# The first layer's attention tiles written out, each with its own order of scores, products, sums and x

## The chip, the cores and the metric

One core of a Trainium2 chip. The metric is device time in microseconds of one execution; lower is better. The engines: TensorE (PE: matmuls and transposes, with its weight loads as PEld), VectorE (DVE), ScalarE (ACT), GpSimd (POOL) and SyncE (SP), on whose queue all of this kernel's loads and stores are issued.

## What is computed

```python
# q, k, v: (B=4, H=8, S=576, D=64), float32
q_d, k_d, v_d = (t.reshape(B, H, 144, 4, D).mean(axis=3) for t in (q, k, v))
out_up = np.repeat(softmax(scale * q_d @ k_d.T) @ v_d, 4, axis=2)
mask = np.abs(pos[:, None] - pos[None, :]) < 4
out_local = softmax(np.where(mask, scale * q @ k.T, -1e9)) @ v
x = (out_up + out_local) as (B * S = 2304, H * D = 512)
h = x @ w_in                          # first layer, 512 -> 2048 -> 512
x = (h * sigmoid(h)) @ w_out
r = np.maximum(x @ w2_in, 0)          # second layer, same sizes
return (s * r * r + b) @ w2_out
```

Each query sees seven keys locally, and 144 pooled keys.

## The kernel before

**Tiles.** Every matmul of the two layers is made of three, of the high and low parts of both operands. The first layer goes over N1 = 8 tiles of T1 = 288 rows (half a batch each). Tile t has 32 blocks of 12 matmuls: "up" f (512 to 128 of the 2048 columns) and "down" f. They are dealt out in 8 slots of 4 blocks (48 matmuls, counted as places k = 0 to 47). Slot 0 has up 0, up 1, up 2, down 0; slot u has up 2u+1, down 2u-1, up 2u+2, down 2u; slot 7 has up 15, down 13, 14, 15. Behind an up block stand ACT's tanh (L880), VectorE's gate (L1152), ACT's high part (L836) and GpSimd's low part (`g_low`, L320). Down f waits for the low part of f.

**Attention beside it.** During tile t the attention of the half that tile t+1 needs is prepared; tile 0 and the time ahead of it work otherwise and are not changed. A unit is one head of one half: 8 per half. TensorE puts a unit's parts between its blocks: scores (L587, L590; the local ones and the pooled ones), transposes of the pooled probabilities `prob_d` (L614), and the matmuls on the pooled values (`attend`, L635). Between these stand VectorE's `maxima` (L1081, L1084), ACT's `exps` (L844, and a copy of the local scores into `s_sb`), VectorE's `normalise` (L1103 to L1107) and `pT_copy` (L1122), and ACT's `evacuate`. GpSimd makes the pooled keys (`qk_sums`, L1436 and L1440) and the pooled values (`v_sums`, L1451 and L1455), both once for two units. In SyncE's queue, per unit: `load_qk` and `load_v` for later units, `read_band` of the unit before, and `store_band`, which waits for the unit's exps. Before each tile stand the windows of v (`load_windows`, four transfers), which wait for the last sum of the tile before.

**Local part by rows.** The stored bands of a half's 8 units come back as rows of seven scores (`e_rows`). In the softmax slot VectorE and ACT make `p_rows` of them. Then for each of 9 groups of rows a product with the windows of v goes into one of two buffers (`weigh`: GpSimd L1497, and VectorE L1263 for i = 2, 5, 8), and VectorE reduces it (`sum_row`, L1273). Product i waits for sum i-2, by these lines:

```python
if not (isinstance(n, int) and n < 2):
    gp.wait_ge(rows_summed, n - 1)
```

Three sums at a time are transposed on TensorE (`turn`, L677), and ACT copies them (`place`). When the third turn is placed, VectorE adds the pooled part for each of four chunks (`x_add`, L1283), ACT rounds (`x_round`) and GpSimd takes the rest (`x_low`); the next tile's up 0 waits for each chunk (`x1_ready`). The local scores, the transposes and the turns share two banks of PSUM with what ACT evacuates.

**Order.** All orders are written by hand in the tables at the top and in each engine's `slot_rows`. `UNITS` says which unit's scores are in which slot, as a count on from the half's first: the lead is 7 units in tiles 2 to 6, while tile 1 makes 14 units (two in each of slots 0 to 5). Tiles 2 to 5 are a loop (`Fori`, two turns of two tiles) on every engine; tiles 1, 6 and 7 are straight code. In tile 6 only the half's last unit is left to finish. Tile 7 has no attention, and the second layer follows.

## Time and profile before

| | |
|---|---|
| median of three runs | 1015.57 us (1011.75 to 1016.58) |
| the profiled execution | 1015.92 us, its span 1014.1 us |
| mean granted clock of TensorE | 0.981 |
| TensorE busy | 956.6 us, 94% of the span |
| VectorE, ACT, GpSimd busy | 474.0, 365.2, 431.7 us |
| tiles 1 to 6 of the first layer | from 113.9 to 563.5 us of the span |
| tile 7 and the second layer | from 563.5 us on |

The span is from the first to the last instruction of one profiled execution. A busy TensorE is not TensorE at its peak: matmuls overlap, their ends are modelled, and they take twice as long where the granted clock is half. The clock's column is 1.00 at 2.4 GHz and 0.50 at 1.2 GHz. Idle time of another engine costs nothing unless TensorE waits for it.

### The profile page before, as it was taken

Reading aid. Unit: us, or ns where it says so; the run is one execution under the profiler, and the core shown is the slowest. Engines: PE = TensorE matmul, PEld = TensorE weight load, DVE = VectorE, ACT = ScalarE, POOL = GpSimd, SP = SyncE. Lnnn points to the kernel's source line nnn. Section 1 sums busy time; section 2 is a strip of 40 time slices with the busy share of each in tenths; the row PEclk is TensorE's granted clock in tenths of the full one; section 3 lists DMA queues with packets and bytes.
Section 4 is the critical chain, followed back from the end, with each engine's and each line's share of the span. In section 5 each row is a group of like instructions: output and inputs, shape, how many; then the busy total and the mean of one; then the engine's idle time right before and its main releaser. Section 6 shows DMA issues by size and latency. Waiting matters only on the chain.

```text
span 1014.1 us, 16827 instructions
## 1 busy us (share of the span) xinstructions
PE 956.6 (94%) x6071; PEld 874.1 (86%) x6071; DVE 474.0 (47%) x975; ACT 365.2 (36%) x951; POOL 431.7 (43%) x426
## 2 busy tenths in 40 slices
PE   8999997788998978998999999999999999999998
PEld 8899987777988977998999998888888888888897
DVE  5577434656747726647638465223222322322232
ACT  5665432232343332443333564223222322322232
POOL 6678355645555645555646322221322222222222
PEclk9899999889999989999999999999999999999999
DMA  6555444133152142152130554002000200100010
GB/s 184 156 166 144 101 108 102 29 79 98 45 117 65 41 108 71 45 133 48 41 73 1 158 167 131 8 1 73 11 0 1 83 0 0 62 0 0 0 43 22
DMA packets 87179, 68.85 MB, mean 68 GB/s; under 512 B 38720, under 2 KB 73024, under 8 KB 87104
## 3 DMA queue, kind: packets, MB, share of 16 engines
q1 hardware_dynamic: 87104, 67.86, 25.0%
q8 instruction: 46, 0.75, 0.3%
q14 instruction: 29, 0.24, 0.1%
HBM read 52.76 MB, written 15.08 MB: 67 GB/s over the span
## 4 chain that ended last, share of the span: by engine, by line
PE 65%; issue 13%; POOL 11%; DVE 6%; ACT 2%; DMA 1%; POOLq 0%; SPq 0%; ACTq 0%; DVEq 0%
PE pH L797 19%; PE pY L812 19%; PE pH L737 11%; PE pY L742 8%; POOL weighted L1497 3%; POOL g_hl L320 3%; PE pS L587 2%; POOL vd_f L1451 2%; POOL pair L1436 1%; POOL x_hl L320 1%; DMA stage_in<-w_in 1%; PE pS L590 1%; DVE act L1152 1%; DVE g_gap L1273 1%; PE pO L641 1%
## 5 line engine op out<-in xcount | busy, mean ns | idle before, releaser
L320 POOL TENSOR_TENSOR g_hl<-act,g_hl 128x288 fp32r<-128x288 f32 (+2 forms) x208 | 203.0, 976 | 504.5 <-ACT g_hl L836 504.5
L737 PE MATMUL pH<-x_hl,w_in_hl 128*128 128x288 f32 x1518 | 250.2, 306 | 11.4 <-POOL x_hl L320 5.0
L742 PE MATMUL pY<-g_hl,w_out_hl 128*128 128x288 f32 x1536 | 249.4, 302 | 2.2 <-POOL g_hl L320 2.2
L737 PEld LDWEIGHTS pH<-x_hl,w_in_hl 128*128 128x128 f32 x1518 | 216.8, 193 | 15.9 <-POOL x_hl L320 8.6
L742 PEld LDWEIGHTS pY<-g_hl,w_out_hl 128*128 128x128 f32 x1536 | 216.1, 190 | 3.6 <-POOL g_hl L320 3.6
L797 PE MATMUL pH<-x_hl,w_in_hl 128*128 128x512 f32 (+1 forms) x960 | 208.4, 368 | 0.0
L812 PE MATMUL pY<-w_out_hl,g_hl 128*128 128x512 f32 x864 | 207.8, 390 | 0.0
L797 PEld LDWEIGHTS pH<-x_hl,w_in_hl 128*128 128x128 f32 x960 | 169.0, 188 | 31.0
L812 PEld LDWEIGHTS pY<-w_out_hl,g_hl 128*128 128x128 f32 x864 | 161.2, 188 | 33.2 <-POOL g_hl L320 0.3
L836 ACT ACTIVATE g_hl<-act 128x288 fp32r<-128x288 f32 (+2 forms) x208 | 104.1, 500 | 229.1 <-DVE act L1152 125.3
L1384 DVE TENSOR_TENSOR act<-act 128x512 f32<-128x512 f32 (+1 forms) x80 | 55.5, 694 | 270.6 <-ACT act L1056 270.6
L1056 ACT ACTIVATE act<-pH 128x512 f32<-128x512 f32 (+1 forms) x80 | 44.3, 554 | 166.0 <-PE pH L797 165.7
L880 ACT ACTIVATE act<-pH 128x288 f32<-128x288 f32 x128 | 52.1, 407 | 135.9 <-PE pH L737 135.8
L1152 DVE SCALAR_TENSOR_TENSOR act<-act,pH 128x288 f32<-128x288 f32 x128 | 57.4, 448 | 63.0 <-ACT act L880 62.1
L1497 POOL TENSOR_TENSOR weighted<-p_rows,v_loc 128x896 f32<-128x896 f32 x36 | 60.8, 1689 | 23.0 <-DVE p_rows L1254 18.0
L1273 DVE TENSOR_REDUCE g_gap<-weighted 128x128 f32<-128x896 f32 x36 | 63.3, 1760 | 11.4 <-POOL weighted L1497 11.0
L587 PE MATMUL pS<-qk_f 128*96 128x102 f32 x360 | 45.3, 264 | 7.0 <-POOL d_f L1440 7.0
L587 PEld LDWEIGHTS pS<-qk_f 128*96 128x96 f32 x360 | 41.5, 174 | 8.8 <-POOL d_f L1440 8.8
L1451 POOL TENSOR_TENSOR vd_f<-vd_f 72x512 f32<-72x512 f32 x32 | 40.8, 1275 | 18.2 <-DMA vd_f<-vp 18.2
L844 ACT ACTIVATE pS<-pS,stats 72x144 f32<-72x144 f32 x60 | 20.8, 346 | 68.6 <-DVE stats L1084 52.6
L1386 DVE TENSOR_SCALAR act<-act,sb_col 128x512 f32<-128x512 f32 (+1 forms) x80 | 41.6, 520 | 2.9
L614 PE MATMUL pO<-ident,prob_d 72*72 72x72 f32 x120 | 18.9, 240 | 23.2 <-ACT g_gap L836 12.4
(141 smaller groups left out, 821.1 us busy)
## 6 DMA issues: line engine op xcount, KB each, us to landing
qk_f<-qk SPq DMA_DIRECT2D x32, 292.0 KB, 3.5
vd_f<-vp SPq DMA_DIRECT2D x64, 144.0 KB
stage_in<-w_in SPq DMA_DIRECT2D x32, 256.0 KB, 2.9
stage_out<-w_out SPq DMA_DIRECT2D x32, 256.0 KB, 3.0
v_loc<-vp SPq DMA_DIRECT2D x24, 240.0 KB, 4.9
score_bands<-act SPq DMA_DIRECT2D x48, 114.8 KB, 2.5
qk_f<-qk SPq DMA_DIRECT2D x64, 72.0 KB, 3.0
x_scratch<-y_sb SPq DMA_DIRECT2D x8, 576.0 KB, 4.8
```

What stands on the lines that cost most here:

```text
L320: eng.tensor_tensor(lo, full, hi.bitcast(F32), ALU.subtract).then_inc(signal, 1)
L587: pe.matmul(work(n).s_loc[:, j, :], qk_f[:, buf, q0:q0 + TQ], qk_f[:, buf, c:c + KW], start=not masked_by_pe(n) and j == 0, stop=True, ski ...
L737: last = pe.matmul(pH[:, f % 2, 0:T1], w_in[:, wp, c, f * P:(f + 1) * P], x1[:, par, mp, c, :], start=c + n == 0, stop=c == C - 1 and n == 2)
L742: last = pe.matmul(pY[:, c, 0:T1], w_out[:, wp, f, c * P:(c + 1) * P], g_hl[:, f % RING, mp, 0:T1], start=f + n == 0, stop=f == NF - 1 and ...
L797: last = pe.matmul(pH[:, f % 2, 0:T], w_in[:, wp, c, f * P:(f + 1) * P], x2_hl[:, xp, c, 0:T], start=c + n == 0, stop=c == C - 1 and n == 2)
L812: last = pe.matmul(pY[:, j, :], g_hl[:, f % RING, gp, j * P:(j + 1) * P], w_out[:, wp, f, :], start=f + n == 0, stop=f == NF - 1 and n == 2)
L836: return sc.activation(dst, src, ACT.Copy)
L1152: ve.scalar_tensor_tensor(act1[:, f % RING, :], act1[:, f % RING, :], 1.0, pH[:, f % 2, 0:T1], ALU.add, ALU.mult).then_inc(L[0].g_ready, 1)
L1273: ve.tensor_reduce(o_row[i].rearrange("p (h d) -> p h d", h=2), weighted[:, i % 2].rearrange("p (h r d) -> p h d r", h=2, r=NR), AX.X, ALU ...
L1384: ve.tensor_tensor(g, g, g, ALU.mult).then_inc(squared, 1)
L1451: gp.tensor_tensor(src[:, :, 0:2, :], src[:, :, 0:2, :], src[:, :, 2:4, :], ALU.add).then_inc(vpair_summed, 1)
L1497: gp.tensor_tensor(*weigh_operands(i), ALU.mult).then_inc(weighed_by_pool, 1)
```

## The change

The loop over tiles 2 to 5 is gone: tiles 1 to 6 are written out on all engines, and tables give tiles 1 and 2 orders of their own. Tile 1 makes units 1 to 12 (two in each of slots 0 to 3), tile 2 makes 5 to 14 (two in slots 0 and 1); from tile 3 on it is 7 to 14, as before. All nine products of a tile are on GpSimd. Sums, counted by slot in `SUM`, are no longer in the slots of their products: one stands at the head of a slot, the others at its end. In GpSimd's slots two products stand ahead of everything else (in the softmax slot they stand behind), the key sums stand behind the first low part of the slot, and the value sums behind them. In slots with two units, maxima stand ahead of the gate, and exps ahead of the high part. The last turn is at place 6 of slot 7 instead of 14 (tile 1: two turns in slot 7, at 6 and 47). In slot 7 `x_add` 0 is ahead of the gate and the rounding of x ahead of the unit's exps. TensorE waits for the copies of turns (`bank_placed`) ahead of the transposes also, and a turn waits for what holds the bank at its place.

```diff
@@ -53,18 +53,21 @@
 LEAD = 7
 UNITS = [(u + LEAD,) for u in range(H)]
-FIRST_UNITS = [(1, 2), (3, 4), (5, 6), (7, 8), (9, 10), (11, 12), (13,), (14,)]
-
+UNITS_IN = {1: [(1, 2), (3, 4), (5, 6), (7, 8), (9,), (10,), (11,), (12,)],
+            2: [(5, 6), (7, 8), (9,), (10,), (11,), (12,), (13,), (14,)]}
+
+SOFTMAX, SOFTMAX_IN = 2, {1: 5, 2: 3}
 WEIGH = {2: (0, 1), 3: (2, 3), 4: (4, 5), 5: (6, 7), 6: (8,)}
-FIRST_WEIGH = {5: (0, 1, 2), 6: (3, 4, 5), 7: (6, 7, 8)}
-BY_VECTOR = (2, 5, 8)
-BY_POOL = tuple(i for i in range(TB) if i not in BY_VECTOR)
+WEIGH_IN = {1: {5: (0, 1, 2), 6: (3, 4, 5), 7: (6, 7, 8)}, 2: {3: (0, 1), 4: (2, 3, 4), 5: (5, 6), 6: (7, 8)}}
+SUM = {2: (0,), 3: (1, 2), 4: (3, 4), 5: (5, 6), 6: (7, 8)}
+SUM_IN = {1: {5: (0, 1), 6: (2, 3, 4, 5), 7: (6, 7, 8)}, 2: {3: (0,), 4: (1, 2), 5: (3, 4, 5), 6: (6, 7, 8)}}
+QK_AHEAD = {(1, 9): 0, (2, 9): 0, (1, 12): 2}
 GROUP = 3
-TURNS = {(4, 24): 0, (6, 24): 1, (7, 14): 2}
-FIRST_TURNS = {(6, 24): 0, (7, 12): 1, (7, 42): 2}
-
-ONE_UNIT, LAST_UNIT, FIRST_LAST_UNIT = (9, 15, 38), (3, 20, 38), (3, 18, 47)
-TWO_UNITS = (3, 7, 19), (27, 31, 43)
+TURNS = {(4, 24): 0, (6, 24): 1, (7, 6): 2}
+TURNS_IN = {1: {(6, 24): 0, (7, 6): 1, (7, 47): 2}, 2: {(5, 24): 0, (6, 24): 1, (7, 6): 2}}
+
+ONE_UNIT, LAST_UNIT, FIRST_LAST_UNIT = (9, 15, 38), (18, 22, 40), (18, 22, 36)
+TWO_UNITS = (4, 7, 20), (28, 31, 44)
...
@@ -468,21 +471,22 @@
                     sp.wait_ge(wout_ready, NF)
                     load_windows((2, 0, 1))
-                def tile1(t, h, following):
-                    ahead = 3 if isinstance(t, int) and t == 1 else 1
+                def tile1(t, following):
+                    h = prepared(t)
                     for u in range(H):
-                        for k in units(t, u):
-                            if ahead == 1 or len(units(t, u)) == 1:
+                        now = units(t, u)
+                        for k in now:
+                            if len(now) == 1:
+                                if w := unit(h, k + QK_AHEAD.get((t, k), 1)):
+                                    load_qk(w)
                                 if w := unit(h, k + 1):
-                                    if k != FIRST_UNITS[-2][0] or ahead == 1:
-                                        load_qk(w)
                                     load_v(w)
                             if w := unit(h, k - 1):
                                 read_band(w)
                             if w := unit(h, k):
                                 store_band(w)
-                            if ahead == 3 and len(units(t, u)) == 2:
-                                load_qk(unit(h, k + 3))
+                            if len(now) == 2 and (w := unit(h, k + 3)):
+                                load_qk(w)
                                 load_v(unit(h, k + 1))
                         if u == 1:
...
                     last.then_inc(rows_turned, 1)
-                def placed(t, u, k):
-
-                    before = [g for (slot, at), g in turns(t).items() if slot == u and at < k]
-                    if before:
-                        pe.wait_ge(rows_placed, TB // GROUP * (t - 1) + max(before) + 1)
+                def bank_placed(t, u, k):
+
+                    before = [g for (slot, at), g in turns(t).items() if (slot, at) < (u, k)]
+                    if t > 1 or before:
+                        pe.wait_ge(rows_placed, TB // GROUP * (t - 1) + len(before))
                 def small_rows(t, h, u, k):
...
@@ -691,17 +688,27 @@
                     elif u < H - 1:
                         places = ONE_UNIT,
                     else:
-                        places = (FIRST_LAST_UNIT if isinstance(t, int) and t == 1 else LAST_UNIT),
+                        places = (FIRST_LAST_UNIT if late(t, u) else LAST_UNIT),
                     for v, (at_trans, at_scores, at_attend) in zip(now, places):
-                        if k == at_trans:
-                            trans_unit(unit(h, v - 1))
+                        before = unit(h, v - 1)
+                        if k == at_trans and before:
+                            bank_placed(t, u, k)
+                            trans_unit(before)
                         if k == at_scores:
                             score_unit(unit(h, v))
                         if (u, k) in turns(t):
-                            turn(t, turns(t)[u, k], unit(h, v - 1))
-                        if k == at_attend and unit(h, v - 1):
-                            placed(t, u, k)
-                            attend_unit(unit(h, v - 1))
+                            if not before:
+                                pe.wait_ge(o_copied, H * (HALVES - 1))
+                            elif k < at_trans:
+                                pe.wait_ge(o_copied, before[0] - H)
+                            elif k < at_attend:
+                                pe.wait_ge(pT_copied, before[0] + 1)
+                            else:
+                                pe.wait_ge(o_copied, before[0] - H + 1)
+                            turn(t, turns(t)[u, k])
+                        if k == at_attend and before:
+                            bank_placed(t, u, k)
+                            attend_unit(before)
                 def up1(t, par, f, c, fill=False):
                     if fill and c == 0:
@@ -778,11 +785,8 @@
                     if u < H - 1:
                         keep_warm(WARM_SOFTMAX)
                 tile1(0, 0, (1, 1, 0), fill=True, rows=False)
-                tile1(1, 1, (2, 0, 1))
-                with pe.Fori(0, B - 2) as i:
-                    tile1(2 * i + 2, 0, halves(i, 0))
-                    tile1(2 * i + 3, 1, halves(i, 1))
-                tile1(N1 - 2, 0, (HALVES - 1, 1, B - 1))
+                for t in range(1, N1 - 1):
+                    tile1(t, t % 2, prepared(t))
                 tile1(N1 - 1, 1, None)
...
@@ -967,38 +971,44 @@
                 def slot_rows(t, h, u):
                     now = units(t, u)
-                    last = u == H - 1
                     here = groups(t, u)
-                    if w := unit(h, now[0] - 2):
+                    two = len(now) == 2
+                    if (w := unit(h, now[0] - 2)) and not (u == 0 and late(t - 1, H - 1)):
                         evacuate(w)
                     if u == 1:
                         tanh1(t, CARRIED)
                         g_high(L[0], t, CARRIED, 2, T1)
+                    if u == H - 1:
+                        place(t, h, here[0])
                     if u == 0:
                         y_out1(t - 1)
                     f, more = UPS[u][0], UPS[u][1:]
                     tanh1(t, f)
-                    if last:
-                        place(t, h, here[0])
+                    if two:
+                        exps(unit(h, now[0]))
+                    if u == H - 1 and not late(t, u):
+                        x_round(t, h, 0)
                     g_high(L[0], t, f, 2, T1)
                     if u == softmax_in(t):
                         row_exps(t, h)
-                    if w := unit(h, now[0]):
+                    if u == H - 1 and not late(t, u):
+                        for c in range(1, C):
+                            x_round(t, h, c)
+                    if two:
+                        evacuate(unit(h, now[0] - 1))
+                    elif w := unit(h, now[0]):
                         exps(w)
-                    if len(now) == 2:
-                        evacuate(unit(h, now[0] - 1)) if now[0] > 0 else None
-                    if not last:
+                    if u < H - 1:
                         for g in here:
                             place(t, h, g)
-                    if last and len(here) == 1:
-                        for c in range(C):
-                            x_round(t, h, c)
                     for f in more:
                         tanh1(t, f)
+                    if two:
+                        exps(unit(h, now[1]))
+                    for f in more:
                         g_high(L[0], t, f, 2, T1)
-                    if len(now) == 2:
-                        exps(unit(h, now[1]))
...
                 def sum_row(t, i):
-                    if i in BY_VECTOR:
-                        weigh(t, i)
-                        ve.wait_ge(weighed_by_vector, len(BY_VECTOR) * (t - 1) + BY_VECTOR.index(i) + 1)
-                    else:
-                        ve.wait_ge(weighed_by_pool, len(BY_POOL) * (t - 1) + BY_POOL.index(i) + 1)
-                    if not (isinstance(t, int) and t == 1):
+                    ve.wait_ge(weighed, TB * (t - 1) + i + 1)
+                    if t > 1 and i == 0:
                         ve.wait_ge(rows_turned, TB // GROUP * (t - 1))
                     ve.tensor_reduce(o_row[i].rearrange("p (h d) -> p h d", h=2),
                                      weighted[:, i % 2].rearrange("p (h r d) -> p h d r", h=2, r=NR), AX.X,
...
@@ -1285,38 +1280,44 @@
                 def slot_rows(t, h, u):
                     now = units(t, u)
-                    last = u == H - 1
-                    weighs = weigh_in(t, u)
+                    sums = sum_in(t, u)
+                    two = len(now) == 2
+                    finish = u == H - 1 and not late(t, u)
                     if u == 1:
                         gate1(t, CARRIED)
+                    at_once = 0 if u == softmax_in(t) else 1
+                    for i in sums[:at_once]:
+                        sum_row(t, i)
+                    if finish:
+                        x_add(t, h, 0)
+                        gate1(t, UPS[u][0])
                     if w := unit(h, now[0] - 1):
                         pT_copy(w)
-                    f, more = UPS[u][0], UPS[u][1:]
-                    gate1(t, f)
+                    if two:
+                        maxima(unit(h, now[0]))
+                    if not finish:
+                        gate1(t, UPS[u][0])
                     if u == softmax_in(t):
                         row_normalise(t, h)
-                    if last and len(groups(t, u)) == 1:
-                        for c in range(C):
+                    if finish:
+                        for c in range(1, C):
                             x_add(t, h, c)
-                    if w := unit(h, now[0]):
+                    if not two and (w := unit(h, now[0])):
                         maxima(w)
-                    for i in weighs[:1]:
-                        sum_row(t, i)
                     if w := unit(h, now[0]):
                         normalise(w)
-                    if len(now) == 2:
+                    if two:
                         pT_copy(unit(h, now[0]))
-                    for f in more:
+                        maxima(unit(h, now[1]))
+                    for f in UPS[u][1:]:
                         gate1(t, f)
-                    if len(now) == 2:
-                        maxima(unit(h, now[1]))
-                    for i in weighs[1:]:
+                    if two:
+                        normalise(unit(h, now[1]))
+                    for i in sums[at_once:]:
                         sum_row(t, i)
-                    if len(now) == 2:
-                        normalise(unit(h, now[1]))
                     if u == softmax_in(t) - 1:
                         row_shift(t, h)
-                    if last and len(groups(t, u)) == 2:
+                    if late(t, u):
                         for c in range(C):
                             x_add(t, h, c)
...
@@ -1502,30 +1502,31 @@
                 def slot_rows(t, h, u):
                     now = units(t, u)
-                    last = u == H - 1
-                    weighs = [i for i in weigh_in(t, u) if i in BY_POOL]
+                    two = len(now) == 2
                     if u == 1:
                         g_low(L[0], t, CARRIED, T1)
-                    if len(now) == 2:
+                    if two:
                         qk_sums(unit(h, now[1]))
-                    elif w := unit(h, now[0]):
+                    softmax = u == softmax_in(t)
+                    for i in weigh_in(t, u)[:0 if softmax else 2]:
+                        weigh(t, i)
+                    g_low(L[0], t, UPS[u][0], T1)
+                    if not two and (w := unit(h, now[0] + 1)):
+                        qk_sums(w)
+                    if not two and (w := unit(h, now[0])):
                         v_sums(w)
-                    for i in weighs[:1]:
-                        weigh(t, i)
-                    f, more = UPS[u][0], UPS[u][1:]
-                    g_low(L[0], t, f, T1)
-                    for i in weighs[1:]:
-                        weigh(t, i)
-                    if last and len(groups(t, u)) == 1:
+                    if u == H - 1 and not late(t, u):
                         for c in range(C):
                             x_low(t, h, c)
-                    for f in more:
+                    for i in weigh_in(t, u)[:1 if softmax else 0]:
+                        weigh(t, i)
+                    for f in UPS[u][1:]:
                         g_low(L[0], t, f, T1)
-                    if len(now) == 2:
+                    if two:
                         v_sums(unit(h, now[1]))
-                    elif w := unit(h, now[0] + 1):
-                        qk_sums(w)
-                    if last and len(groups(t, u)) == 2:
+                    for i in weigh_in(t, u)[1 if softmax else 2:]:
```

## Rows read from the trace of the kernel before

**Rows 1.** Tiles 1 to 6: length, busy PE, PEld, DVE, ACT, POOL; clock, DMA.

```profile
113.90:213.50 99.60, 80.93 (x591) 76.69 (x589) 49.47 (x124) 30.95 (x96) 49.34 (x50) 0.92 0.37 85
213.50:286.10 72.60, 66.64 (x505) 64.50 (x505) 44.34 (x88) 26.91 (x77) 41.56 (x43) 0.97 0.28 70
286.10:358.50 72.40, 65.42 (x505) 62.88 (x505) 44.01 (x87) 27.39 (x80) 42.23 (x44) 1.00 0.34 80
358.50:436.70 78.20, 68.33 (x506) 66.25 (x506) 44.01 (x87) 25.73 (x74) 40.45 (x42) 0.93 0.29 71
436.70:508.20 71.50, 65.34 (x505) 62.86 (x506) 44.00 (x87) 26.60 (x77) 41.39 (x43) 1.00 0.33 79
508.20:563.50 55.30, 55.06 (x416) 54.36 (x417) 33.58 (x46) 19.84 (x50) 28.86 (x28) 1.00 0.14 32
```

**Rows 2.** TensorE's waits: us in total, times, longest us.

```profile
PE pO L614 <- ACT g_gap L836: 12.4, 12, 1.9
PE pO L614 <- DVE prob_d L1107: 10.8, 10, 4.4
...
PE pO L677 <- DVE pdT L1122: 2.4, 1, 2.4
```

**Rows 3.** Timeline of TensorE in tile 5: start, us, instructions, idle before.

```profile
453.36 1.49 PE L737 MATMUL pH<-x_hl,w_in_hl 128*128 128x288 f32 x10
...
461.11 1.48 PE L737 MATMUL pH<-x_hl,w_in_hl 128*128 128x288 f32 x10
...
481.80 1.49 PE L737 MATMUL pH<-x_hl,w_in_hl 128*128 128x288 f32 x10
```

**Rows 4.** Timeline of TensorE: the last turn of tile 1; head of tile 4.

```profile
210.18 0.41 PE L677 MATMUL pO<-ident,act 128*128 128x128 f32 x2 [3.62 <-DVE o_last L1273]
...
363.74 0.85 PE L737 MATMUL pH<-x_hl,w_in_hl 128*128 128x288 f32 x2 [3.90 <-issue]
```

**Rows 5.** Timeline of tile 1, TensorE and SyncE's queue.

```profile
119.79 0.78 PE L737 MATMUL pH<-x_hl,w_in_hl 128*128 128x288 f32 x4
...
124.35 0.78 PE L737 MATMUL pH<-x_hl,w_in_hl 128*128 128x288 f32 x4
...
150.03 0.32 SPq L442 DMA_DIRECT2D score_bands<-act  x1
...
159.28 0.64 PE L635 MATMUL pO<-pdT,vd_sum 72*128 72x72 f32 x4
...
166.46 0.32 PE L614 MATMUL pO<-ident,prob_d 72*72 72x72 f32 x2 [0.46 <-DVE prob_d L1107]
```

**Rows 6.** Products (L1263, L1497), reductions (L1273): ns min/median/max.

```profile
L1263 DVE TENSOR_TENSOR weighted<-p_rows,v_loc x18: 1079/1377/3610, 182.9 to 553.0; 128x896 f32<-128x896 f32 x18
...
L1497 POOL TENSOR_TENSOR weighted<-p_rows,v_loc x36: 1683/1690/1696, 171.8 to 549.2; 128x896 f32<-128x896 f32 x36
...
L1273 DVE TENSOR_REDUCE g_gap<-weighted x36: 1681/1774/1803, 173.6 to 545.7; 128x128 f32<-128x896 f32 x36
```

**Rows 7.** Timeline of tile 5, GpSimd's first product and VectorE's first.

```profile
458.28 1.69 POOL L1497 TENSOR_TENSOR weighted<-p_rows,v_loc 128x896 f32<-128x896 f32 x1 [4.43 <-DVE p_rows L1254]
...
467.83 3.60 DVE L1263 TENSOR_TENSOR weighted<-p_rows,v_loc 128x896 f32<-128x896 f32 x1
```

**Rows 8.** Groups of GpSimd from 278 to 345 us: busy us, mean ns.

```profile
L320 POOL TENSOR_TENSOR g_hl<-act,g_hl 128x288 fp32r<-128x288 f32 x15 | 12.7, 846 | 17.5 <-ACT g_hl L836 17.5
...
L1451 POOL TENSOR_TENSOR vd_f<-vd_f 72x512 f32<-72x512 f32 x4 | 5.1, 1275 | 0.0
...
L1455 POOL TENSOR_TENSOR vd_sum<-vd_f 72x256 f32<-72x256 f32 x4 | 3.0, 758 | 0.3
L1440 POOL TENSOR_TENSOR d_f<-pair 128x290 f32<-128x290 f32 x4 | 2.7, 670 | 0.6 <-POOL pair L1436 0.5
```

**Rows 9.** Timeline around tile 5's head: a band, and unit 8's key sums.

```profile
435.46 0.32 SPq L442 DMA_DIRECT2D score_bands<-act  x1
...
445.53 1.15 POOL L1436 TENSOR_TENSOR pair<-qk_f 128x580 f32<-128x580 f32 x1 [0.49 <-DMA qk_f<-qk]
```

77 lines of the change are left out of this document (29 added, 48 removed).

## The prediction

> **What bounds the kernel now.** I read the windows by tile first. A tile of the first layer is 384 matmuls of 288 columns, plus the attention work of the next half. Tile 6, which has next to no attention work left, takes 55.3 us; tiles 2, 3 and 5 take 71.5 to 72.6, tile 4 takes 78.2 and tile 1 takes 99.6 [rows 1]. TensorE is busy 94% of the whole span, so the second layer and tile 7 (nothing of them is changed) have no room. What counts is what TensorE waits for in tiles 1 to 6, 449.6 us by the sum of the six windows.
>
> The waits of TensorE give the names: the transposes of prob_d wait for ACT (which clears the bank they write) and for VectorE (which makes prob_d) [rows 2]. Such waits sum to less than is lost, because a long one also brings the granted clock down: tile 1, with waits of 2.4 and 4.4 us [rows 2], ran at a mean of 0.92, tile 4 at 0.93, and tiles 3 and 5, which have none over 1.9, at 1.00 [rows 1]. Below 1.00 means that part of the tile ran at 1.2 instead of 2.4 GHz.
>
> The timeline of TensorE gives the price of undisturbed work. Slot 2 of tile 5 goes from 453.36 to 461.11: 7.75 us with one unit. Slots 3 and 4, to 481.80, take 20.69 together instead of 15.5 and a turn [rows 3]. A turn is some 0.35 us (two of its three transposes: 0.41) [rows 4]. So an undisturbed tile with eight units would be 8 x 7.75 + 3 x 0.35 = 63.1 us; tile 5 loses 8.4, of which 4.8 in slots 3 and 4. A slot with two units is 2 x 4.56 = 9.12 us, as 119.79 to 124.35 is half of one [rows 5]. Tile 1 has six such slots now: 54.7 + 15.5 + 1.1 = 71.3 undisturbed; it loses 28.
>
> **Part 1: the loop is written out.** Where the loop turns back (head of tile 4) TensorE stops for 3.90 us for "issue" [rows 4]. Tile 4 against the mean of tiles 3 and 5: 78.2 - 71.95 = 6.2 us, the slow clock behind the stop included. Tiles 3 and 5, inside the loop, have the same loads at their heads and no such stop. I take -6.2; bounds 0 (the fetch is late for the loads' sake) and -6.2. The Trainium skill (Runtime: NRT & Kernel Launch, Instruction fetch mechanics) says that a taken branch to outside the window of pages waits for the fetch, while straight code hides it. By that rule it is -6.2 too again; but the second layer's loops jump back too, and the trace lists no issue wait of TensorE there, so a jump alone may cost 0.
>
> **Part 2: VectorE loses its three products a tile.** There they take 1.08 to 3.61 us each, median 1.38; on GpSimd a product takes 1.69, with next to no spread [rows 6]. The one at 467.83 ran beside GpSimd's for 3.60 us [rows 7], and behind it on VectorE stood a reduction, the normalising of the scores and a gate: that is slot 4's loss. Slot 3's is a reduction (1.76) that stood between maxima and normalise in slot 2, so that prob_d, a gate, ACT's high part and ACT's evacuation were late in turn, and key sums that stood behind two products. The new order has the reductions first or last in a slot and the key sums ahead of the products. I count both losses as gone, -4.8, and 0.9 of smaller ones of the same kind in slots 5 and 6.
> GpSimd pays. Slots 3 to 5 have two products there (3.4), two low parts (1.6) and half the key and value sums (1.15 + 0.67 + 1.28 + 0.76, halved, is 1.9) [rows 8, 9], with gaps 7.0 of 7.75 us. Following the new order on from 461.11: block 7's low part is done 7 us into slot 3 and needed 1.8 into slot 4, block 9's 6 into slot 4 and needed 1.8 into slot 5. GpSimd keeps up, by 2 to 3 us.
> The last turn moves from place 14 to place 6 of slot 7; sum 8 is done 0 to 0.5 us after it is wanted: +0.3. The rounding of x goes ahead of the exps of slot 7, and the next tile's head, where I put 2.1 of tile 5's loss, then loses 0.7 (low parts of x behind value sums on GpSimd).
>
> **Part 3: a new wait at the heads of tiles 3 to 5.** In slot 0 the key sums of unit 8 stood behind both low parts; now they stand between them. Their load stands on SyncE's queue behind the band of unit 14 and the windows of v: the band is issued at 435.46, and the pair sum starts when the load has landed, at 445.53 [rows 9]. That is 10.1 us after the band and 9.0 after the tile's head. In the new slot 7 unit 14's exps go behind the four x_adds and roundings, so the band leaves about 0.4 us ahead of the next head instead of 1.1: landing at +9.7. Pair, d_f and the gap between them add 2.0, block 1's low part 0.8: ready at +12.5. TensorE wants it at block 1's down matmuls, slot 0 (8.4) + 1.7 = +10.1. So a wait of 2.4 us where there was none; everything of TensorE stands behind it, and the clock may fall (tile 4's 6.2 less its stop of 3.9 is 2.3, the most that I would give that; I take 1.0). Bounds: 0 (landing 2.4 sooner) and 5.
> Tiles 3, 4 and 5 are then 63.1 + 0.3 + 0.7 + 2.4 + 1.0 = 67.5 each: 202.5 against 222.1, **-19.6**, part 1 included.
>
> **Part 4: tile 1.** Its slots have 2,2,2,2,1,1,1,1 units, twelve instead of fourteen. Slots 0 to 4 now end at 165.9 (the transposes three matmuls into slot 5 start at 166.46): 52.0 us [rows 5]. Each double slot has two short waits for prob_d, since maxima stood behind a gate and exps behind a high part. Both go 0.9 us earlier, more than the waits. Late next is the value sum, whose load is issued behind the band: from the band (150.03) to the first matmul on the sum (159.28) are 9.2 us [rows 5]. The new band is 4.0 us into its slot and the sum wanted 3.3 into the next, 8.4 later: 0.8 for one slot, 1.8 in all, as each wait gives the next slot time. New: 4 x 9.12 + 1.8 + 7.75 = 46.1, **-5.9**.
> Slots 5 to 7 took 47.6. In tile 5 the first product starts 4.9 us after its slot's head (458.28) [rows 7]; here the value sums stand ahead, so 6.2. From there product and reduction follow one another: sums 0, 1 and 2 are done 9.7, 12.2 and 14.0 us after slot 5's head, and TensorE wants sum 2 and the copy behind it at 12.0 for the first turn: wait 2.3. Slot 6 has four sums among its other work: sum 5 done at 23 to 24, wanted at 19 to 21: wait 3 to 4. Sum 8 done at 32.3 to 34.2, wanted at 30.5 to 33.4: wait 1 to 2. From the last turn to tile 2's first matmul are 3.3 us [rows 1, 4], in part filled now; then the turn is the tile's last work, and they are empty. Tile 2 starts 38.4 after slot 5, the slow clock counted: **-9.2**. Bounds 33 (each sum a little sooner) and 44.
>
> **Part 5: tile 2** has ten units instead of eight: 65.8 undisturbed. Its head keeps 2.7 of slow clock and waits for x; the double slots' value sums cost 1.8. Product 6 stands ahead of block 11's low part and waits for sum 4, which comes behind slot 5's last gate: block 11's down matmuls are 1.9 late. Sum 8 is 0.9 late. Total 73.1 against 72.6: **+0.5**, bounds -5 and +5. Tile 6: -0.3.
>
> **Sum.** -19.6 - 5.9 - 9.2 + 0.5 - 0.3 = -34.5. The profiled execution took 1015.92 (span 1014.1 and 1.8 around it), 0.35 above the median of 1015.57. 1015.9 - 34.5 = 981.4; I say **981**.
>
> **Rivals.** (a) As above: 981, own range 970 to 990, chance 0.52; that the loop's stop stays where it was (987) is in it. (b) The new waits are hidden: the keys land in time (-3.4 in each of three tiles) and tile 1's chain is shorter (-5): 966, chance 0.22. Against it speaks that the windows of v stand ahead of this load. (c) GpSimd becomes the bound: 7.0 of 7.75 us leaves no room, and five tiles lose 3 us more: 996, chance 0.19. For it: one low part behind two products has to wait 3.4 us. (d) Slower: GpSimd and VectorE exclude one another, so products and reductions no longer overlap. GpSimd has 41.4 us of work in tile 5 [rows 1], 46.5 with three more products; nine reductions of 1.76 on top are 62.3 of 63.1 us, and slots 3 to 5 then hold 7.0 + 3.5 of 7.75, so that TensorE waits 2.75 in each: 8.2 a tile, twice that in tiles 1 and 2, 57 in all, 1038. It decides from 7 us a tile on (34.5 over five tiles). Against: GpSimd's products keep to 1.70 and the reductions to 1.80 [rows 6]. Chance 0.05, no change 0.02. The Trainium skill (SBUF — State Buffer, Who interferes with whom) says that only VectorE instructions with two SBUF inputs, or in some faster modes, exclude GpSimd, and a reduction never. By that rule (d) is out, and the trace agrees.
>
> So faster 0.94, same 0.02, slower 0.04; 0.5% (5 us) is about what a measurement of this kernel can tell from no change. The range that leaves out 2 in 10 goes from (b)'s lower side, 961, to (c), 998.
>
> **What would show it.** Tile 1 near 84.5, tile 2 near 73, tiles 3 to 5 alike and near 67.5, tile 6 near 55. No issue wait. The waits of transposes for ACT gone. A wait of 2 to 3 us of pY for g_hl 10 us into tiles 3, 4 and 5, with the pair sum waiting for qk_f. In tile 1, turns that wait 2 to 4 us for reductions. The prediction is wrong if low parts are late in slots 3 to 6, if the reductions are not at 1.76, or if tile 4 differs from 3 and 5.

## The result and the profile after

The changed kernel takes 969.12 us (median of four runs, 966.73 to 970.30) against 1013.66 of the kernel before in the same runs: ratio 0.9557, 95% interval 0.952 to 0.9594. The forecast was 981, with 961 to 998 as its range. The profiled execution's span went from 1014.1 to 967.1 us, the mean granted clock from 0.981 to 0.993.

The windows by tile, each from TensorE's first matmul of the tile to that of the next (length; busy time of PE, PEld, DVE, ACT, POOL; granted clock, DMA), answer to [rows 1]:

```profile
113.66:196.14 82.48, 71.29 (x564) 69.79 (x562) 44.27 (x109) 28.02 (x89) 49.47 (x49) 0.97 0.42 99
196.14:268.16 72.02, 69.18 (x533) 68.16 (x534) 40.26 (x97) 28.79 (x88) 50.24 (x50) 0.96 0.33 78
268.16:333.13 64.97, 64.20 (x507) 62.94 (x506) 36.88 (x84) 26.41 (x78) 46.38 (x46) 1.00 0.37 87
333.13:397.28 64.15, 63.91 (x506) 62.90 (x506) 36.91 (x84) 26.38 (x78) 46.38 (x46) 1.00 0.37 88
397.28:461.95 64.67, 64.21 (x506) 62.96 (x506) 36.89 (x84) 26.43 (x78) 46.34 (x46) 1.00 0.38 87
461.95:517.31 55.36, 54.88 (x414) 53.96 (x414) 28.13 (x43) 20.36 (x51) 32.10 (x31) 1.00 0.12 30
```

| tile | before | forecast | after |
|---|---|---|---|
| 1 | 99.6 | 84.5 | 82.5 |
| 2 | 72.6 | 73.1 | 72.0 |
| 3 | 72.4 | 67.5 | 65.0 |
| 4 | 78.2 | 67.5 | 64.1 |
| 5 | 71.5 | 67.5 | 64.7 |
| 6 | 54.9 | 55.0 | 55.4 |

(Tile 6 of before is cut at TensorE's first matmul of tile 7 here, at 563.15; the prediction had 563.5.) The six tiles went from 449.25 to 403.65 us, 45.6 less, which is the whole difference of the spans (47.0) but 1.4 us. The forecast was 34.5 less. The 11 us between are 8.7 in tiles 3 to 5, 2.0 in tile 1, 1.1 in tile 2 and -0.7 in tile 6.

TensorE's waits over the span (total, times, longest) answer to [rows 2]:

```profile
PE pO L674 <- DVE o_last L1268: 4.2, 3, 2.5
PE pY L749 <- POOL g_hl L316: 3.5, 5, 1.4
PE pO L674 <- DVE g_gap L1268: 3.3, 1, 3.3
PE pH L744 <- POOL x_hl L316: 2.9, 1, 2.9
PE pO L674 <- DVE pdT L1129: 2.5, 1, 2.5
```

The transposes (L615 now) wait for nobody any more, the scores neither, and there is no issue wait. Most of what is left are the turns (L674) and the head of tile 2, nearly all at tile 1, where they were forecast: 2.5, 3.3 and 2.5 us for the turns and 2.9 for the head. The rest of the turns' waits is 1.45 in tile 2 and 0.3 in tile 6; the waits for low parts (`pY <- g_hl`) are 1.39 in tile 2, 0.53 in tile 3 and 0.25 in tile 5, and the others lie behind tile 6.

The clock stands at 1.00 in tiles 3 to 5, so the slow stretch of 1.0 us a tile that part 3 allowed is not there. The reason is at the tile's head. Lines of the timeline of tile 4's head answer to [rows 9], first from SyncE's queue (SPq), then GpSimd, then TensorE:

```profile
330.85 0.32 SPq L445 DMA_DIRECT2D score_bands<-act  x1
333.13 1.15 SPq L389 DMA_DIRECT2D qk_f<-qk  x2
...
340.41 1.15 POOL L1434 TENSOR_TENSOR pair<-qk_f 128x580 f32<-128x580 f32 x1 [1.94 <-DMA qk_f<-qk]
341.64 0.67 POOL L1438 TENSOR_TENSOR d_f<-pair 128x290 f32<-128x290 f32 x1
...
333.13 2.59 PE L744 MATMUL pH<-x_hl,w_in_hl 128*128 128x288 f32 x10
...
343.75 0.69 PE L749 MATMUL pY<-g_hl,w_out_hl 128*128 128x288 f32 x4
```

GpSimd does wait for the keys, 1.94 us, but they land 7.3 us after the tile's head (333.13), not 9.7, because the band of unit 14 (330.85) leaves 2.3 us ahead of the head and not 0.4. From band to pair sum are 9.6 us here, 10.9 in tile 3 and 10.6 in tile 5, around the 10.1 of [rows 9]. Block 1's low part is done in time for the matmuls at 343.75. In tiles 3 and 5, where the keys took longer behind a band that left as early, it is 0.53 and 0.25 us late.

### The profile page after: what moved, and what is told of

The parts are those of the page before. It is cut to its first block, busy times and chain, and to the rows that moved or that the text cites. A ratio compares the mean times of both kernels' runs of the same rounds, so it can differ in the third digit from the quotient of the medians.

```text
span 967.1 us, 15804 instructions
## 1 busy us (share of the span) xinstructions
PE 942.9 (97%) x6071; PEld 868.0 (90%) x6071; DVE 438.4 (45%) x957; ACT 363.3 (38%) x951; POOL 458.9 (47%) x444
## 4 chain that ended last, share of the span: by engine, by line
PE 82%; POOL 7%; issue 5%; DVE 4%; ACT 1%; DMA 0%; SPq 0%; POOLq 0%; ACTq 0%; DVEq 0%
PE pH L801 20%; PE pY L816 20%; PE pH L744 16%; PE pY L749 14%; PE pS L588 3%; POOL weighted L1495 2%; PE pO L636 2%; POOL g_hl L316 1%; POOL x_hl L316 1%; PE pS L591 1%; PE pO L642 1%; POOL vd_f L1449 1%; PE pY L762 1%; PE pO L615 1%; DVE act L1159 1%
## 5 line engine op out<-in xcount | busy, mean ns | idle before, releaser
L744 PE MATMUL pH<-x_hl,w_in_hl 128*128 128x288 f32 x1518 | 245.4, 303 | 4.9 <-POOL x_hl L316 2.9
L749 PE MATMUL pY<-g_hl,w_out_hl 128*128 128x288 f32 x1536 | 246.2, 300 | 3.5 <-POOL g_hl L316 3.5
L749 PEld LDWEIGHTS pY<-g_hl,w_out_hl 128*128 128x128 f32 x1536 | 213.9, 189 | 4.7 <-POOL g_hl L316 4.7
L1495 POOL TENSOR_TENSOR weighted<-p_rows,v_loc 128x896 f32<-128x896 f32 x54 | 90.6, 1690 | 7.8 <-DVE g_gap L1268 5.2
L588 PE MATMUL pS<-qk_f 128*96 128x102 f32 x360 | 43.0, 256 | 0.0
L1434 POOL TENSOR_TENSOR pair<-qk_f 128x580 f32<-128x580 f32 x31 | 36.2, 1166 | 10.7 <-DMA qk_f<-qk 8.6
L1129 DVE COPY pdT<-pO 72x144 f32<-72x144 f32 x48 | 14.5, 301 | 49.2 <-PE pO L615 49.0
```

The source lines that it names most:

```text
L588: pe.matmul(work(n).s_loc[:, j, :], qk_f[:, buf, q0:q0 + TQ], qk_f[:, buf, c:c + KW], start=not masked_by_pe(n) and j == 0, stop=True, ski ...
L744: last = pe.matmul(pH[:, f % 2, 0:T1], w_in[:, wp, c, f * P:(f + 1) * P], x1[:, par, mp, c, :], start=c + n == 0, stop=c == C - 1 and n == 2)
L749: last = pe.matmul(pY[:, c, 0:T1], w_out[:, wp, f, c * P:(c + 1) * P], g_hl[:, f % RING, mp, 0:T1], start=f + n == 0, stop=f == NF - 1 and ...
L1495: gp.tensor_tensor(weighted[:, i % 2].rearrange("p (h r d) -> p h r d", h=2, r=NR), p_rows[:, i, :].rearrange("p (h r) -> p h r", r=NR).un ...
```

## Experiments

Ratios are to the kernel before, measured beside it, with their 95% intervals in brackets. Tile times are the windows of one profiled execution each, and executions of one kernel differ by some us: the kernel before took 1009.9 to 1017.1 us beside the first four runs.

**e1_written_out.** The kernel before with this edit, on all five engines:

```diff
-                tile1(1, 1, (2, 0, 1))
-                with pe.Fori(0, B - 2) as i:
-                    tile1(2 * i + 2, 0, halves(i, 0))
-                    tile1(2 * i + 3, 1, halves(i, 1))
-                tile1(N1 - 2, 0, (HALVES - 1, 1, B - 1))
+                for t in range(1, N1 - 1):
+                    tile1(t, t % 2, prepared(t))
```

> The kernel before with tiles 2 to 5 written out and nothing else changed. If the stop at tile 4's head came from the loop's jump, it goes with the slow stretch behind it: 6.2 us less (ratio 0.994), tile 4 then like tiles 3 and 5 at 71.5 to 72.5 us, no issue wait. If it came from the loads at a tile's head, the wait stays or shows at other heads: ratio 1.00.

Measured: 0.9917 (0.9899 to 0.9935). Tile 4 takes what its neighbours take, at clock 1.00:

```profile
283.49:355.14 71.65, 65.57 (x505) 62.86 (x506) 43.66 (x87) 26.43 (x76) 41.33 (x43) 1.00 0.34 79
355.14:426.46 71.32, 65.32 (x505) 62.88 (x506) 43.98 (x87) 26.52 (x76) 41.33 (x43) 1.00 0.34 79
426.46:497.96 71.50, 65.44 (x505) 62.88 (x506) 43.98 (x87) 26.54 (x76) 41.35 (x43) 1.00 0.33 79
```

The stop was the loop's: the loads at the heads are the same and none waits for issue. Tile 4 gives 6.9 us, tile 1 1.5, tile 2 0.3 and tile 3 0.8. That a branch waits for its target's instructions is the rule of the Trainium skill that the prediction named (Runtime: NRT & Kernel Launch, Instruction fetch mechanics). The run agrees with it for this loop, but no run separates the fetch from what else the turn of a loop costs.

**e2_products_moved and e12_sums_last.** The kernel before, loop and all, with `BY_VECTOR = ()`; then the first reduction of a one-unit slot moved to the slot's end as well:

```diff
-BY_VECTOR = (2, 5, 8)
+BY_VECTOR = ()
...
-                    for i in weighs[:1]:
+                    for i in weighs[:1] if len(now) == 2 else ():
                         sum_row(t, i)
...
-                    for i in weighs[1:]:
+                    for i in weighs[1:] if len(now) == 2 else weighs:
                         sum_row(t, i)
```

> The kernel before with all nine products on GpSimd, in the old places and the old order. If the products on VectorE are what costs, tiles 2, 3 and 5 get 2 to 3 us shorter and the whole 8 to 12 us (ratio 0.990). If the order does it (the reduction between maxima and normalise, the key sums behind the products), they stay within 1 us, and the wait for d_f grows, since the key sums then stand behind as many products or more: ratio 1.00 or above.

> e2_products_moved (the kernel before with all products on GpSimd) with one edit on VectorE: in slots with one unit the first reduction no longer stands between maxima and normalise but last in the slot. In e2_products_moved tile 5's slot 3 takes 10.51 us against 7.75 undisturbed, with a wait of 0.88 for ACT's evacuation and one of 1.46 for the key sums. If that reduction delays the evacuation, the first wait goes and the second stays or grows, since the key sums stand behind the same two products: 0.9 to 1.5 us less in each of tiles 2 to 5, 4 to 6 us in all (ratio 0.978). If both waits are the key sums' doing, nothing changes (ratio 0.9835).

Measured: 0.9835 (0.9812 to 0.9859), and 0.9792 (0.9768 to 0.9817). Tiles 2 to 5 are 2.3 to 2.6 us shorter each, as the first theory had it, and tile 1 3.9, so that the whole gains more than its 8 to 12 us. TensorE's timeline of tile 5 (heads of slots 3, 4 and 5, and the waits between) in e2_products_moved:

```profile
451.15 1.48 PE L737 MATMUL pH<-x_hl,w_in_hl 128*128 128x288 f32 x10
...
453.51 0.32 PE L614 MATMUL pO<-ident,prob_d 72*72 72x72 f32 x2 [0.88 <-ACT g_gap L836]
...
456.13 0.77 PE L587 MATMUL pS<-qk_f 128*96 128x102 f32 x6 [1.46 <-POOL d_f L1440]
...
461.66 1.48 PE L737 MATMUL pH<-x_hl,w_in_hl 128*128 128x288 f32 x10
...
470.14 1.49 PE L737 MATMUL pH<-x_hl,w_in_hl 128*128 128x288 f32 x10
```

and in e12_sums_last, of the same slots:

```profile
442.77 1.49 PE L737 MATMUL pH<-x_hl,w_in_hl 128*128 128x288 f32 x10
...
446.72 0.77 PE L587 MATMUL pS<-qk_f 128*96 128x102 f32 x6 [1.50 <-POOL d_f L1440]
...
452.25 1.49 PE L737 MATMUL pH<-x_hl,w_in_hl 128*128 128x288 f32 x10
...
460.32 1.48 PE L737 MATMUL pH<-x_hl,w_in_hl 128*128 128x288 f32 x10
```

With the products gone, slot 4 takes 8.5 us instead of 10.2, and slot 3 keeps its 10.5: wait 0.88 for ACT, 1.46 for the key sums, both as long as in the kernel before. With the reduction last, the wait for ACT goes and the one for the key sums stays, at 1.50; slot 3 takes 9.5 and slot 4 8.1. So the three causes that the prediction named for these two slots are each there: taking the product away gives 1.7 us, the reduction's new place 1.0 in slot 3 and 0.4 in slot 4. The key sums' 1.5 is read from the wait; no run moves them alone. In e12_sums_last tiles 2 to 5 are 1.9 to 2.8 us shorter than in e2_products_moved, more than the 0.9 to 1.5 expected, and tile 1 is 2.2 longer, so that the whole comes out as expected.

**e3_products_back.** The changed kernel, products 2, 5 and 8 on VectorE again:

```diff
                 def sum_row(t, i):
-                    ve.wait_ge(weighed, TB * (t - 1) + i + 1)
+                    if i in BY_VECTOR:
...
+                        ve.tensor_tensor(weighted[:, i % 2]..., ALU.mult).then_inc(weighed_by_vector, 1)
```

> The changed kernel with products 2, 5 and 8 back on VectorE, each just ahead of its reduction, all else as changed. If the order does it, this is within 5 us of the changed kernel in all (ratio 0.957 to 0.961), with the loss in tile 1, where VectorE's chain sets the turns (3 products of 1.1 to 1.7 us: +3 to +5). If moving the products was worth much by itself, every tile gets 2 to 3 us longer: ratio 0.97.

Measured: 0.969 (0.9665 to 0.9715), 985.87 us: 1.3% of the time of before is lost again, some 13.5 us. The whole is what the second theory had, though with 5.6 and 5.7 us in tiles 2 and 3 where it had 2 to 3; tile 1 is 2.3 us longer and tiles 4 and 5 2.8 and 2.3. (The profiled execution, 990.56 us, was the longest of the four.) The waits show how:

```profile
PE pO L677 <- DVE o_last L1282: 10.0, 6, 3.1
PE pO L677 <- DVE pdT L1132: 8.2, 5, 3.6
PE pY L752 <- POOL g_hl L319: 6.5, 4, 2.9
```

The last turn now waits in every tile (six times, up to 3.1), and so does the turn that stands behind a copy of VectorE in tiles 1 to 5. Tiles 2 and 3 lose most, since a low part is 2.1 and 2.9 us late there too. My reading is that the new order has a reduction and the copy in one row ahead of each turn, with no room for a product. So the new order is worth less with the products on VectorE.

**e4_leads_back.** The changed kernel with the units shared out as before:

```diff
-UNITS_IN = {1: [(1, 2), (3, 4), (5, 6), (7, 8), (9,), (10,), (11,), (12,)],
-            2: [(5, 6), (7, 8), (9,), (10,), (11,), (12,), (13,), (14,)]}
+UNITS_IN = {1: [(1, 2), (3, 4), (5, 6), (7, 8), (9, 10), (11, 12), (13,), (14,)]}
```

with tile 2's other tables left out, so that it has the later tiles'.

> The changed kernel with the units shared out as before: tile 1 makes 14 (two in slots 0 to 5), tile 2 the eight of every later tile, with their softmax, products, sums and turns in the later tiles' slots. The work is the same. If the shape of tiles 1 and 2 is a good part of the gain, tile 1 goes from 82.5 to 88 to 92 us (2.8 more of work, and the chain of sums in slots 5 to 7 against more other work of VectorE), tile 2 from 72.0 to about 66: together +2 to +4, ratio 0.959. If the lead of two tiles matters more, the turns of tile 1 wait longer, +8 or more: ratio 0.964.

Measured: 0.9531 (0.9515 to 0.9547), no slower than the change.

```profile
112.97:202.37 89.40, 75.68 (x591) 73.92 (x590) 47.13 (x121) 29.53 (x97) 53.19 (x53) 0.96 0.42 96
202.37:268.39 66.02, 66.02 (x505) 65.44 (x506) 37.06 (x85) 27.43 (x80) 46.62 (x46) 0.95 0.32 77
```

Tiles 1 and 2 take 89.4 + 66.0 = 155.4 us, against 82.5 + 72.0 = 154.5. The lead over two tiles moves 6 to 7 us of work and waits from tile 1 to tile 2 and is worth at most 1; the gain of the two tiles (17.7, or 16.8 in this run) comes without it, from the new order with the moved products and, for some 2 us by e1_written_out, the written-out loop.

**e5_round_behind and e6_keys_behind.** The changed kernel with ACT's roundings behind the exps again; and with slot 0's key sums behind the second low part:

```diff
                     elif w := unit(h, now[0]):
                         exps(w)
+                    if u == H - 1 and not late(t, u):
+                        for c in range(C):
+                            x_round(t, h, c)
...
-                    if not two and (w := unit(h, now[0] + 1)):
+                    if not two and u and (w := unit(h, now[0] + 1)):
                         qk_sums(w)
...
+                    if not two and u == 0 and (w := unit(h, now[0] + 1)):
+                        qk_sums(w)
```

> The changed kernel with ACT's four roundings of x behind the unit's exps again in slot 7 of tiles 2 to 6. The four low parts of x start about 2 us later, and each of four or five heads waits 1 to 2 us: +4 to +8 us in all. The band leaves at most 1 us earlier, which gives back the 0.3 to 0.6 that two heads wait for the key sums. If the heads have slack, no change.

> The changed kernel with the key sums of slot 0 behind the second low part again, in tiles 3 to 6. The wait of block 1's down matmuls in tiles 3 and 5 (0.5 and 0.25 us) goes: 0 to -1.5 us in all. As the prediction had it (2.4 us and a slow clock in each of three tiles) it would be -10; the profile after already speaks against that.

Measured: 0.9542 (0.9512 to 0.9572) and 0.9562 (0.9529 to 0.9595), both the same as the change. Tiles 3 to 5 take 64.9, 64.6 and 64.2 with the roundings behind, so that their new place is worth nothing. GpSimd, which makes the low parts behind them, is busy with the value sums until then: ahead of tile 4 the roundings end at 330.4 and the value sums at 330.5. With the key sums behind, tiles 3 to 5 take 64.2 each; that is the 0.5 to 0.8 us by which tiles 3 and 5 were longer than tile 4, too little to see in the whole.

**e7_collide and e9_keys_first.** Was the new wait of part 3 a wrong mechanism or a wrong size? The x_adds (L1278 after) of tile 3 and those of tile 5 before (L1283), with min/median/max in ns:

```profile
L1278 DVE TENSOR_TENSOR x_rows<-x_rows,g_gap x4: 443/448/457, 327.3 to 329.1; 128x288 f32<-128x288 f32 x4
```

```profile
L1283 DVE TENSOR_TENSOR x_rows<-x_rows,g_gap x4: 446/1057/1078, 502.2 to 505.2; 128x288 f32<-128x288 f32 x4
```

Before, the first began with GpSimd's value sums under way, and three of the four took 1.06 us beside GpSimd's instructions; the last, with GpSimd idle, took 0.45. After, GpSimd was idle when they began. The edits, the second on top of the first (it also takes the load and e7_collide the value sums out of their old places):

```diff
+                    early = u == H - 1 and t > 2
+                    if early and (w := unit(h, now[0])):
+                        gp.wait_ge(rows_placed, TB // GROUP * t)
+                        v_sums(w)
                     g_low(L[0], t, UPS[u][0], T1)
...
+                    if following and t > 1 and (w := unit(following, LEAD + 1)):
+                        load_qk(w)
                     if following:
                         sp.wait_ge(rows_summed, TB * t)
                         load_windows(following)
```

> The changed kernel, but in slot 7 of tiles 3 to 6 GpSimd makes the value sums at the moment when VectorE's x_adds start (it waits for the last placed turn), ahead of block 15's low part. If the four x_adds took 0.39 to 0.46 us in the changed kernel only because no GpSimd instruction was under way when they began, they take 0.8 to 1.1 here as in the kernel before, the last unit's band leaves 1.5 us or more later, unit 8's keys land later by as much, and block 1's down matmuls wait 1.5 to 2.5 us in each of tiles 3 to 5: the wait that was forecast, +4 to +8 us. If the x_adds keep to 0.4, nothing changes.

> e7_collide with one more edit: from tile 3 on the load of unit 8's keys stands ahead of the windows of v on SyncE's queue, instead of behind them. In e7_collide tiles 4 and 5 take 67.8 and 68.2 us, with waits of about 3 us for block 1's low part. If these come from the keys landing late behind band and windows, they go: tiles 4 and 5 at 64 to 65 us, ratio 0.953 to 0.956. If they come from anything else that the collision shifts (the band itself, the low part of block 15), they stay at 68.

Measured: 0.961 (0.9572 to 0.9648), and 0.9507 (0.9491 to 0.9524). Lines of e7_collide's timeline at the end of tile 4, with tile 5's head at 399.97: VectorE, GpSimd, the band, and the key sums:

```profile
395.21 0.93 DVE L1278 TENSOR_TENSOR x_rows<-x_rows,g_gap 128x288 f32<-128x288 f32 x1
396.06 2.04 DVE L1278 TENSOR_TENSOR x_rows<-x_rows,o_up_last 128x288 f32<-128x288 f32 x2
...
395.90 0.84 POOL L1453 TENSOR_TENSOR vd_sum<-vd_f 72x256 f32<-72x256 f32 x1
...
399.35 0.32 SPq L445 DMA_DIRECT2D score_bands<-act  x1
...
410.25 1.15 POOL L1434 TENSOR_TENSOR pair<-qk_f 128x580 f32<-128x580 f32 x1 [6.00 <-DMA qk_f<-qk]
```

The windows of tiles 4 and 5, first of e7_collide, then of e9_keys_first:

```profile
332.14:399.97 67.83, 64.90 (x507) 64.45 (x506) 38.52 (x85) 26.50 (x78) 46.52 (x46) 0.97 0.35 83
399.97:468.13 68.16, 64.93 (x508) 64.48 (x507) 38.53 (x85) 26.51 (x78) 46.53 (x46) 0.97 0.35 83
```

```profile
330.43:393.49 63.06, 63.06 (x507) 62.83 (x506) 38.85 (x85) 26.57 (x78) 46.63 (x46) 1.00 0.37 89
393.49:456.56 63.07, 63.07 (x508) 62.85 (x506) 38.52 (x85) 26.59 (x78) 46.60 (x46) 1.00 0.37 90
```

Three of the x_adds take 0.93 to 1.06 us, the band leaves 0.6 us ahead of the head (forecast: 0.4), the keys land at +10.3 (forecast: 9.7), and block 1's low part is 2.9 and 3.2 us late in tiles 4 and 5 (forecast: 2.4). These tiles take 67.8 and 68.2 us at a clock of 0.97 (forecast: 67.5). That the whole is so near the forecast is in part luck: the wait is longer, but the head, which was to lose 0.7, loses nothing, because the value sums no longer stand ahead of the low parts of x. With the keys' load ahead of the windows, all that TensorE lost goes: 63.1, undisturbed, in spite of the collision. So the mechanism of part 3 is shown, and so is the term that was wrong in it.

The Trainium skill (SBUF — State Buffer, SBUF: two separate sides) says that a VectorE instruction with two SBUF inputs and a GpSimd instruction that reads SBUF exclude each other: the one that starts first has the shared ports for the whole instruction. The x_adds, 0.45 alone and 1.06 beside GpSimd, agree.

**e8_softmax_earlier, e10_both_earlier and e11_x_low_first.** One on top of the other, from the changed kernel. First tile 1's softmax in slot 4; then tile 2 with the later tiles' tables, and e6's edit; then the low parts of x ahead of the value sums:

```diff
-SOFTMAX, SOFTMAX_IN = 2, {1: 5, 2: 3}
+SOFTMAX, SOFTMAX_IN = 2, {1: 4, 2: 3}
-WEIGH_IN = {1: {5: (0, 1, 2), 6: (3, 4, 5), 7: (6, 7, 8)}, ...
+WEIGH_IN = {1: {4: (0, 1), 5: (2, 3), 6: (4, 5, 6), 7: (7, 8)}, ...
-SUM_IN = {1: {5: (0, 1), 6: (2, 3, 4, 5), 7: (6, 7, 8)}, ...
+SUM_IN = {1: {4: (0,), 5: (1, 2), 6: (3, 4, 5), 7: (6, 7, 8)}, ...
...
+                    if u == H - 1 and not late(t, u):
+                        for c in range(C):
+                            x_low(t, h, c)
                     if not two and (w := unit(h, now[0])):
                         v_sums(w)
```

> The changed kernel with tile 1's softmax in slot 4 instead of 5, products in slots 4 to 7 as 2, 2, 3, 2 and sums as 1, 2, 3, 3. If the chain of sums behind the softmax is what tile 1's turns wait for (2.5, 3.3 and 2.5 us), the first two waits go or halve and tile 1 gets 4 to 7 us shorter, unless VectorE, at slot 3's end, waits for the bands of unit 7 longer than slot 4 can bear: then a wait of 1 to 3 us in slot 4 takes its place. If the waits have another cause, no change.

> e8_softmax_earlier, with tile 2's softmax, products, sums and turns in the slots of the later tiles (softmax in slot 2 instead of 3; it keeps its ten units), and slot 0's key sums behind the second low part as in e6_keys_behind. Tile 2 has a block 1.4 us late for product 6 and a last turn 1.4 us late; both should go: tile 2 from 71.8 to 68 to 69 us, tiles 3 and 5 at 64.2. In all -3.5 to -4.5 against e8_softmax_earlier, ratio 0.946. If VectorE then waits for unit 7's bands at slot 1's end, tile 2 gains nothing.

> e10_both_earlier with GpSimd's four low parts of x ahead of the value sums in slot 7 of tiles 2 to 6. At the heads of tiles 3 to 7 the first ten matmuls take 2.6 us instead of 1.5, while in e7_collide, where GpSimd's low parts of x start 1.2 us earlier against the head, they take 1.5. If the low parts are what the head waits for, each head gives 1.1 us: -4 to -5.5 in all, ratio 0.941. If the value sums are then late for the next slot 0, block 0's low part or the attend there waits and it is less.

Measured: 0.9498 (0.947 to 0.9526), 0.9431 (0.941 to 0.9451) and 0.9407 (0.9378 to 0.9437), the last 953.88 us. Tile 1 of e8_softmax_earlier, tile 2 of e10_both_earlier, tile 3 of e11_x_low_first:

```profile
111.42:188.18 76.76, 69.79 (x563) 68.28 (x562) 44.78 (x109) 27.80 (x89) 49.28 (x49) 0.99 0.45 105
```

```profile
190.75:259.20 68.45, 68.03 (x534) 66.97 (x534) 41.11 (x97) 28.66 (x88) 50.26 (x50) 0.98 0.34 83
```

```profile
259.89:323.00 63.11, 63.11 (x507) 62.74 (x506) 36.92 (x84) 26.41 (x77) 46.43 (x46) 1.00 0.37 90
```

Tile 1 gives 5.7 us: two of its turns now wait 1.3 and 1.8 us, and the first not at all. Tile 2 gives 3.3 (71.8 in e8_softmax_earlier, 68.4 in e10_both_earlier). With the low parts first, the first ten matmuls of a tile take 1.49 us (tile 5's head, below) where they took 2.59:

```profile
386.15 1.49 PE L744 MATMUL pH<-x_hl,w_in_hl 128*128 128x288 f32 x10
```

and tiles 3 to 5 take 63.0 to 63.2 us, which is the 63.1 that the prediction worked out for an undisturbed tile. Only tile 2 loses by that edit, 1.2 us (68.4 to 69.6).

## Why the prediction was right

The direction, the range and the places of the large gains were right; the time was 12 us too high, and some three quarters of that lie in one term. Case (a), which had 0.52, gave itself 970 to 990 us, and 969.12 lies just outside. What came nearest was case (b), the new waits hidden: 966, with 0.22. The keys came in time to within 0.5 us in all three tiles, and tile 1 gave 2.0 us more than forecast, not 5.

- **Undisturbed work, 63.1 us a tile.** Right: e9_keys_first and e11_x_low_first reach 63.0 to 63.2.
- **Part 1, the loop, -6.2.** Right: 8.4 (0.9917) for the whole, 6.9 in tile 4.
- **Part 2, products and reductions, -4.8 and -0.9 a tile.** Right in cause and size: e2 and e12 show the causes, and after the change slots 3 and 4 of tile 4 take 15.8 us together, which is the undisturbed work with its turn. GpSimd has more to do than the 7.0 us a slot that were worked out: it is busy for 6.8, 7.9 and 7.6 us of slots 3 to 5, which last 7.7, 8.1 and 7.7. It keeps up all the same, and no low part is late there: rival (c) is out. Rival (d) too: the products keep to 1.69 and the reductions to 1.77 with half as many again on GpSimd.
- **Part 2, the head of the next tile: 2.1 lost to 0.7.** The step "the rounding of x goes ahead of the exps" failed as a cause. e5_round_behind shows that it does nothing. The head still loses 1.1 us, and e11_x_low_first shows to what: the value sums ahead of the low parts, as the prediction had it. Which edit made 1.1 of the 2.1 no run shows.
- **Part 3, the new wait, 2.4 and 1.0 for the clock.** The mis-sized term is "the band leaves about 0.4 us ahead of the next head". It rested on x_adds of 1.06 us, the size that they had before; they take 0.45, since the same new order took away the GpSimd work that they ran into. The band leaves 2.3 us ahead and the wait is 0 to 0.5. (Before, it left 1.2 us ahead and its keys landed at +8.8 by [rows 1, 9], not 1.1 and +9.0; the +9.7 does not hang on that.) e7_collide gives back the old size and with it tiles of 67.8 and 68.2. Wait and slow clock were put at 10.2 us over three tiles and came to 1.3 (tiles 3 and 5 against tile 4); with the heads 1.2 worse than forecast and the turns 0.9 better, that is 8.7 of the 11 us. The sign "if tile 4 differs from 3 and 5" shows faintly, by 0.5 to 0.8 us, and e6_keys_behind takes it away.
- **Part 4, tile 1, -15.1.** Measured -17.1. Slots 5 to 7 were forecast to take 38.4 us and take 37.9; the turns were to wait 2.3, 3 to 4 and 1 to 2, and from the last turn to tile 2's head were to be 3.3. The turns wait 2.5, 3.3 and 2.5, and the last stretch takes 3.4, of which 2.9 are idle. The other 1.5 us of the difference are in slots 0 to 4, which take 44.6 and not 46.1 (4 x 9.12 + 1.8 + 7.75 is 46.0). The value sums of the double slots were to cost 1.8 there and cost 0.2 in the one place where they are late, 9.2 us behind their band (126.66 to 135.85). The prediction wanted the sum 8.4 us behind the band; in the new slots it is wanted 9.0 behind it. The sharing of units, which the prediction did not price by itself, is worth at most 1 us (e4_leads_back).
- **Part 5, tile 2, +0.5.** Measured -0.6. The two waits that it named, 1.9 for block 11's low part and 0.9 for the last turn, are there with 1.39 and 1.45.

What stays open: why tiles 1 to 3 gain 2.5 us in all when only the loop is written out (the executions of the kernel before differ by more), why the loops of the second layer show no such stop, and which of the moves in slots with two units gives how much of tile 1's first five slots (they were changed together in all runs).

## What to carry to other kernels

Before an instruction's duration goes into a sum for a new order, ask what it ran beside in the old one: the x_adds had two durations, 0.45 and 1.06 us, and the new order picked one. An engine that waits for a load shows the load's name, not what stood ahead of it on its queue; here moving the keys' load ahead of the four transfers of the windows took away all that the collision had cost (67.8 and 68.2 us to 63.1). And when a change moves work between tiles and changes the order within them, try the two apart: here the first was worth at most 1 us.

## What the hardware showed that was not expected

- With VectorE's x_adds back to back and GpSimd idle at their start, GpSimd's low part that began in their midst took 1.48 us instead of 0.80, and the x_adds kept their 0.45:

```profile
328.32 1.18 DVE L1278 TENSOR_TENSOR x_rows<-x_rows,g_gap 128x288 f32<-128x288 f32 x3
328.69 1.48 POOL L316 TENSOR_TENSOR g_hl<-act,g_hl 128x288 fp32r<-128x288 f32 x1 [3.35 <-ACT g_hl L840]
```

- Where GpSimd had begun first, three x_adds took 1.06 and GpSimd's low part 1.08. Who began first decides who pays most.
- GpSimd's products stay within 1.680 to 1.704 us, with 36 or 54 of them, beside reductions or not, in every kernel but e3_products_back. There, with products back on VectorE and the two engines' products side by side, the median is 1.692 but the longest takes 2.47; in the kernel before it was VectorE's that paid, with up to 3.61.
- Not every wait of TensorE of 2 to 3 us is followed by a stretch at 1.2 GHz: behind the first turn of tile 1 (wait of 2.48) the granted clock stays at 1.00 in the 4 us after it, behind the second (3.26) it is 0.76 over the 7 us after. Behind the third (2.51) it is still 1.00 for the first us; then comes the wait of 2.92 at the head of tile 2, and from there it is 0.50 for 3.9 us. Over tiles 3 to 5 no wait exceeded 0.53 and the clock stayed at 1.00.
